# Attention probabilities turned by VectorE and carried through DRAM, instead of turned by TensorE

## The chip, the cores and the metric

The program runs on one core of one Trainium2 chip. The metric is the device time of one execution in microseconds (us), the median of three runs. In this document PE is TensorE (PEld its weight loads), ACT is ScalarE, DVE is VectorE, POOL is GpSimd and SP is SyncE, which does nothing here but issue DMAs.

## The reference

Three layers follow each other on a tensor of 4 batches, 576 tokens and 512 features, all in float32:

```
scores = q @ k.T / 8                      # 4 x 8 heads, 64 features each
keep 32 previous keys (heads 0-3) or every 4th of 128 previous keys (heads 4-7)
attn = exp(scores - max) / (sum + 1e-9);  x = attn @ v
xk, xr = mu * x + (1 - mu) * x_of_the_token_before         # two mixes
x = sigmoid(xr @ w_r) * (relu(xk @ w_k) ** 2 @ w_v)        # 512 -> 1024 -> 512
u = x + (token mix of rank 32 by U and V)
out = u + relu(u @ w_ch1) @ w_ch2                          # 512 -> 2048 -> 512
```

## The kernel before

**Attention in parts and pairs.** The 576 tokens of each batch are cut in two, 256 and 320, which makes eight parts (`k` = 0 to 7, the odd ones with 320 tokens). In each part the eight heads are worked as four pairs (`p` = 0 to 3; pairs 0 and 1 are dilated, 2 and 3 plain). `n = 4k + p` numbers all 32. One pair has four steps:

- A: DVE turns q and k, which DMAs have brought from DRAM, in 32x32 blocks.
- B: PE multiplies q by k into PSUM (L1300, L1313), DVE adds the mask and takes the maximum (L1052 to L1062), ACT takes the exponentials in place in `probs` (L766), four or five units of 64 queries by 64 or 96 keys.
- C: DVE divides by the sum (`normalise`, L1085 to L1090), PE turns the probabilities, one transpose for each unit (L1320), ACT copies the result from PSUM to `probs_t` (L756).
- D: PE multiplies `probs_t` by v (L1331), DVE copies the result into x (L1072 to L1076).

**Beside the second layer.** The second layer is worked in chunks of 256 tokens (`c` = 0 to 8), each chunk in ten slots. A slot is one unit of PE work on the mixed tokens: slots 0 to 3 and 6 to 9 hold the units k0 to k3 and k4 to k7 (12 matmuls of 256 columns), slots 4 and 5 the units r0 and r1 (12 matmuls of 512 columns). ACT takes relu and square of each k unit (`relu` L841, `high_sq` L846), and DVE takes the same square once more and the difference of the two (`square`, L1110 and L1114), because a product is done in three matmuls of high and low parts (L1279 to L1281). The down projection of a unit m, `values(c, m)`, waits for that difference `sq_l`. I call it v0 to v7: v0 in slot 3, v1 in slot 4, v2 in slot 5, v3 in slot 7, v4 in slot 8, and v5, v6 and v7 one after the other in slot 9.

**What sets the order.** Tables (`LATER` and its two relatives) give each step of each pair a slot of this sequence, written out before the run. In the steady state, counted in slots modulo ten, A stands at 3, 5, 8 and 0, B at 4, 6, 9 and 1, C at 8, 0, 3 and 5 and D at 9, 1, 4 and 6, for pairs 0 to 3. The steps of a part stand beside a chunk that is one and a half earlier. The squares are one slot late on DVE. Each engine works in its own order and waits on semaphores. ACT runs the exponentials of a B step one slot after it. The mix of the next chunk (`shift` on ACT, L798 to L807, `mix` on DVE, L1099) stands between them.

**Loads.** SP issues all loads in one order: v of a pair waits until D of the pair three before has run, q and k wait until A of the pair three before has run. In the first parts (`KEYS_BY_SCALAR`, seven pairs) ACT issues k instead of SP. Each of q and k is four DMAs a pair.

Of the kernel before, what the change touches and what calls it, by code (L numbers as in the profile page):

```python
# [21 lines left out]
F32 = mybir.dt.float32  # L22
# [40 lines left out]
KEYS_BY_SCALAR = [(0, 0), (0, 1), (0, 2), (1, 0), (1, 1), (1, 2), (1, 3)]  # L63
# [27 lines left out]

BEFORE = [("B", 0, 0), ("B", 0, 1), ("C", 0, 0), ("B", 0, 2), ("D", 0, 0), ("C", 0, 1), ("B", 0, 3), ("D", 0, 1), ("C", 0, 2),
# [7 lines left out]
SECOND_ONE = {"A": [-5, -4, -2, 0], "B": [-4, -3, -1, 1], "C": [-2, 0, 3, 5], "D": [-1, 1, 4, 6]}  # L100
SLOT_OF = {}
for k in range(1, NPART):
    for p in range(PAIRS):
        for st in "ABCD":
            n = (FIRST_ONE if k == 1 else SECOND_ONE if k == 2 else LATER)[st][p]
            if n is not None:
                SLOT_OF[st, k, p] = NUNIT * (k - 1) + n


def steps_in(slot):  # L110
    return sorted([step for step, n in SLOT_OF.items() if n == slot], key=lambda step: ("ACBD".index(step[0]), step[1:]))

# [69 lines left out]
SCALAR_SQUARES = [0] + list(range(MIX_CHUNK, NC1))  # L182
# [29 lines left out]
def build(nc, q, k_in, v, mu_k, mu_r, w_k, w_v, w_r, u_in, v_in, w_ch1, w_ch2, out):  # L212
    ctx = ExitStack()
    with ctx:
# [24 lines left out]
        probs_t = [sb(f"probs_t{n}", [UK, 5, P], c=first) for n in range(2)]  # L239
        mask_first = sb("mask_first", [P, 2, UK], BF16, c=first)  # L240
# [53 lines left out]
        sb("up_to_wr", [P, WPIECE], c=second)  # L294
# [11 lines left out]


# [22 lines left out]
        normed = sem("normed")  # L330
        carried = sem("carried")
# [113 lines left out]
        for n in range(NPART * PAIRS):  # L445
# [4 lines left out]
            V_COUNT.append(counts[RAWS + n % VALUES])  # L450

# [21 lines left out]
        def _(sp):  # L473
# [99 lines left out]
            for n in range(nth(2, 0), NPART * PAIRS):  # L573
                load_v(*divmod(n, PAIRS))
                if n + 2 < NPART * PAIRS:
                    load_qk(*divmod(n + 2, PAIRS))
                if n == nth(3, 0):
                    load_u()
                    load_piece(PIECE_V)
# [168 lines left out]
        def _(act):  # L748
# [21 lines left out]

            def attention_slot(slot):
# [5 lines left out]
                for k, p in behind:  # L777
                    exps(k, p, 1)

# [130 lines left out]

            def load_keys(k, p, parts=range(4)):
                n = nth(k, p)
                if n >= RAWS:
                    act.wait_ge(turned, n - RAWS + 1)
                for part in parts:
                    act.dma_start(raw_part(k_raw[n % RAWS], k, part), rows_of(k_in, k, p, part)).then_inc(qk_in[n % RAWS], 16)  # L916
# [90 lines left out]
        def _(dve):  # L1007
# [11 lines left out]
            def attention(stage_, k, p):  # L1019
# [23 lines left out]
                elif stage_ == "B":  # L1043

                    if n >= 2:
                        wait_mm(dve, ("C", *divmod(n - 2, PAIRS)))
# [45 lines left out]

            def mix(c, t):
# [12 lines left out]
            def square(c, m):  # L1106

                if c not in SCALAR_SQUARES:
# [3 lines left out]
                wait(dve, square_done, c * M1 + m + 1)  # L1112
# [161 lines left out]
        def _(pe):  # L1274
# [8 lines left out]
            def attention(stage_, k, p):  # L1283
# [37 lines left out]
                else:  # L1321
                    pe.wait_ge(values_in[n % VALUES], V_COUNT[n])
                    wait_drained(pe, ("C", k, p))
                    for i, (query, keys) in enumerate(every):
                        wide = BLOCK if dil and i == 4 else UQ
                        for a in range(UQ // wide):
                            for h in range(2):
                                rows = slice(DH * h, DH * h + DH)
                                block_, first = (4, DH * h + wide * a) if i == 4 else (2 * h + i // 2, UQ * (i % 2))
                                to = query + wide * a  # L1330
                                ins = pe.matmul(run[rows, to:to + wide], v_raw[n % VALUES][0:keys, i + a, rows],  # L1331
                                                probs_t[n % 2][0:keys, block_, first:first + wide], start=True, stop=True)
# [206 lines left out]
```

## Time and profile before

| | us |
|---|---|
| median of three runs | 762.47 (762.42 to 763.02) |
| the profiled execution's own time | 762.07 |
| its span in the profile | 760.0 |
| PE busy | 739.1 (97%) |
| DVE busy | 329.0 (43%) |
| ACT busy | 301.3 (40%) |
| POOL busy | 166.2 (22%) |

The profile is of one execution. Its span goes from the first to the last instruction, and about 2 us of the execution's own time lie around it. A matmul's recorded duration overlaps the next one, so what a group of matmuls costs is read from the starts of the instructions around it. PEclk, the granted clock of TensorE, is at its full value in all slices of the page.

### The profile page before, as it was taken

The numbers are of one execution on the slowest core, as the hardware profiler recorded it, in microseconds if no ns is written. First come the engines' busy times: TensorE is split into PE (matmuls) and PEld (weight loads), VectorE is DVE, ScalarE is ACT, GpSimd is POOL, SyncE is SP. The second block draws the span as 40 slices with busy tenths as digits, with TensorE's granted clock in tenths as the row PEclk, the third lists the DMA queues.
The fourth block names the chain that finished last, engine by engine and source line by source line (L and its number), as shares of the span: only waits on it lengthen the run. The fifth ranks groups of instructions, "written<-read, shape, count | busy, mean of one in ns | idle before, by whom it ended". The sixth has DMA issues, their size and how long they took to land.

```text
span 760.0 us, 13291 instructions
## 1 busy us (share of the span) xinstructions
PE 739.1 (97%) x4960; PEld 647.2 (85%) x4960; DVE 329.0 (43%) x695; ACT 301.3 (40%) x801; POOL 166.2 (22%) x257
## 2 busy tenths in 40 slices
PE   4799999999999999999999999999999999999998
PEld 3678888888888887888899989999999999899997
DVE  6888685868576746635321221312131131213111
ACT  4786767777777656635331111211111111112110
POOL 6897021202121133405871000000000000000000
PEclk9999999999999999999999999999999999999999
DMA  7864443333232101002342102100110210011001
GB/s 143 192 169 87 82 84 55 65 66 59 46 66 51 42 1 56 1 28 74 133 135 34 42 1 41 42 0 16 26 41 0 41 41 0 13 28 41 1 1 41
DMA packets 153746, 39.68 MB, mean 52 GB/s; under 512 B 141536, under 2 KB 147680, under 8 KB 153696
## 3 DMA queue, kind: packets, MB, share of 16 engines
q1 hardware_dynamic: 144000, 37.96, 21.5%
q10 hardware_dynamic: 9696, 1.05, 1.0%
q8 instruction: 31, 0.51, 0.3%
q14 instruction: 19, 0.16, 0.1%
HBM read 30.33 MB, written 4.72 MB: 46 GB/s over the span
## 4 chain that ended last, share of the span: by engine, by line
PE 94%; DVE 2%; ACT 1%; DMA 1%; issue 1%; POOL 0%; ACTq 0%; DVEq 0%
PE bank L1279 29%; PE bank L1281 28%; PE bank L1280 28%; PE bank L1331 3%; PE bank L1300 2%; PE bank L1320 2%; PE bank L1423 1%; PE bank L1435 1%; PE bank L1313 1%; POOL w_l L647 0%; ACTq L916 0%; DMA stage<-in_moe_w_ch_dram 0%; ACT probs L766 0%; DVE probs L1052 0%; DVE q_t L1030 0%
## 5 line engine op out<-in xcount | busy, mean ns | idle before, releaser
L1246 DVE SCALAR_TENSOR_TENSOR h_l<-bank,h_h 128x384 fp32r<-128x384 f32 x96 | 53.5, 558 | 288.1 <-ACT h_h L991 288.1
L991 ACT ACTIVATE h_h<-bank 128x384 fp32r<-128x384 f32 x96 | 47.1, 491 | 312.1 <-PE bank L1281 312.1
L1281 PE MATMUL bank<-ut_h,w_l 128*128 128x384 f32 x384 | 129.4, 337 | 0.0
L1279 PE MATMUL bank<-ut_h,w_h 128*128 128x384 f32 x384 | 129.3, 337 | 0.0
L1280 PE MATMUL bank<-ut_l,w_h 128*128 128x384 f32 x384 | 128.9, 336 | 0.0
L1281 PE MATMUL bank<-w_h,h_l 128*128 128x512 f32 x288 | 113.7, 395 | 0.0
L1280 PE MATMUL bank<-w_l,h_h 128*128 128x512 f32 x288 | 113.5, 394 | 0.0
L1279 PE MATMUL bank<-w_h,h_h 128*128 128x512 f32 x288 | 112.0, 389 | 0.0
L1279 PE MATMUL bank<-xs_h,wk_h 128*128 128x256 f32 x288 | 84.9, 295 | 0.2
L1280 PE MATMUL bank<-xs_l,wk_h 128*128 128x256 f32 x288 | 81.1, 282 | 0.0
L1281 PE MATMUL bank<-xs_h,wk_l 128*128 128x256 f32 x288 | 80.9, 281 | 0.0
L1279 PEld LDWEIGHTS bank<-ut_h,w_h 128*128 128x128 f32 x384 | 72.1, 188 | 4.6 <-issue 0.8
L1280 PEld LDWEIGHTS bank<-ut_l,w_h 128*128 128x128 f32 x384 | 72.1, 188 | 3.6
L1281 PEld LDWEIGHTS bank<-ut_h,w_l 128*128 128x128 f32 x384 | 72.0, 188 | 0.0
L1281 PEld LDWEIGHTS bank<-w_h,h_l 128*128 128x128 f32 x288 | 54.0, 187 | 11.5
L1280 PEld LDWEIGHTS bank<-w_l,h_h 128*128 128x128 f32 x288 | 54.0, 187 | 9.5
L1279 PEld LDWEIGHTS bank<-w_h,h_h 128*128 128x128 f32 x288 | 54.1, 188 | 9.0
L1279 PE MATMUL bank<-wv_h,sq_h 128*128 128x512 f32 x144 | 58.4, 405 | 0.0
L1279 PEld LDWEIGHTS bank<-xs_h,wk_h 128*128 128x128 f32 x288 | 54.8, 190 | 3.9 <-issue 1.4
L1281 PE MATMUL bank<-wv_h,sq_l 128*128 128x512 f32 x144 | 56.9, 395 | 0.0
L1280 PE MATMUL bank<-wv_l,sq_h 128*128 128x512 f32 x144 | 56.9, 395 | 0.0
L1280 PEld LDWEIGHTS bank<-xs_l,wk_h 128*128 128x128 f32 x288 | 54.9, 191 | 1.2
(120 smaller groups left out, 1183.9 us busy)
## 6 DMA issues: line engine op xcount, KB each, us to landing
stage<-in_moe_w_ch_dram SPq DMA_DIRECT2D x16, 512.0 KB, 3.3
out_dram<-result SPq DMA_DIRECT2D x18, 256.0 KB, 2.0
u_tile<-result SPq DMA_DIRECT2D x80, 48.0 KB, 2.0
q_raw<-in_q_dram SPq DMA_DIRECT2D x64, 40.0 KB, 2.1
q_raw<-in_q_dram SPq DMA_DIRECT2D x64, 32.0 KB, 2.0
v_raw<-in_v_dram SPq DMA_DIRECT2D x32, 64.0 KB, 2.4
k_raw<-in_k_dram SPq DMA_DIRECT2D x48, 40.0 KB, 2.1
k_raw<-in_k_dram SPq DMA_DIRECT2D x52, 32.0 KB, 2.0
```

Source lines behind the costliest of these rows:

```text
L991: act.activation(h_h[:, m % KRING, :], h_bank[m % 2][:, 0:C2], ACT.Relu).then_inc(hh_done, 1)
L1246: dve.scalar_tensor_tensor(h_l[:, m % KRING, :], h_bank[m % 2][:, 0:C2], 0.0, h_h[:, m % KRING, :].bitcast(F32), op0=ALU.max, op1=ALU.subt ...
L1279: pe.matmul(dst, lhs[0], rhs[0], start=start, stop=False)
L1280: pe.matmul(dst, lhs[0], rhs[1], start=False, stop=False)
L1281: return pe.matmul(dst, lhs[1], rhs[0], start=False, stop=stop)
L1300: ins = pe.matmul(dst[UQ * a:UQ * a + UQ, h, col:col + keys], q_t[n % 2][rows, query:query + UQ], k_t[p][rows, first_key:first_key + keys] ...
L1313: ins = pe.matmul(out_, q_t[n % 2][rows, query + wide * a:query + wide * a + wide], rhs, start=True, stop=True)
L1320: ins = pe.transpose(run[0:keys, i * P:i * P + P], probs[n % 2][:, keys * i:keys * i + keys], ident[:, :])
L1331: ins = pe.matmul(run[rows, to:to + wide], v_raw[n % VALUES][0:keys, i + a, rows], probs_t[n % 2][0:keys, block_, first:first + wide], sta ...
L1423: pe.matmul(g_bank[b % 2][rows, :].rearrange("p (a b) -> p a b", a=KT), u_pad[:, b % 2, slot, :], xcols(t * P, P), start=slot < 4, stop=sl ...
L1435: ins = pe.matmul(mix_bank[t % 2][:, :], vp[:, col:col + P], g_split[:, b, :], start=n == 0, stop=n == len(parts) - 1)
```

## The change

From pair 2 of part 2 on (n = 10 to 31, 22 pairs) step C is gone from PE and ACT. In its place is a step T, two slots after B. DVE normalises the pair and turns it in 32x32 blocks into a new tile `probs_blocks`; SP writes that tile to DRAM with one DMA and, one slot later, reads it back with one DMA for every 32 keys (two or three), in an order that completes the transpose. D waits for these DMAs and reads `probs_t` in another layout. For the same pairs ACT issues the four DMAs of k, after the second half of the exponentials. In chunks 1 to 6 the squares of units 1, 3, 4 and 6, which DVE took, are taken by ACT. SP's loads are issued slot by slot instead of pair by pair.

```diff
+MOVED_FROM = nth(2, 2)
+KEYS_BY_SCALAR = FIRST_KEYS + [divmod(n, PAIRS) for n in range(MOVED_FROM, NPART * PAIRS)]
@@ the table of slots
+        if nth(k, p) >= MOVED_FROM:
+            del SLOT_OF["C", k, p]
+            SLOT_OF["T", k, p] = SLOT_OF["B", k, p] + 2
-SCALAR_SQUARES = [0] + list(range(MIX_CHUNK, NC1))
+SCALAR_CHUNKS = [0] + list(range(MIX_CHUNK, NC1))
+SCALAR_SQUARES = [(c, m) for c in range(NC1) for m in range(M1) if c in SCALAR_CHUNKS or m in (1, 3, 4, 6)]
@@ SP
+            def probs_to_dram(k, p):
+                n, (nu, keys) = nth(k, p), blocks(k, p)
+                sp.wait_ge(probs_turned, n - MOVED_FROM + 1)
+                wait_mm(sp, ("D", *divmod(n - 2, PAIRS)))
+                sp.dma_start(probs_dram[n % 2][:, 0:nu * keys], probs_blocks[n % 2][:, 0:nu * keys]).then_inc(probs_out, 16)
+
+            def probs_from_dram(k, p):
+                n, (nu, keys) = nth(k, p), blocks(k, p)
+                sp.wait_ge(probs_out, 16 * (n - MOVED_FROM + 1))
+                rows = probs_dram[n % 2][:, 0:nu * keys].rearrange("(g j) (b x) -> b j g x", g=NBLOCK, x=BLOCK * nu)
+                for b in range(keys // BLOCK):
+                    sp.dma_start(moved_view(n, keys)[BLOCK * b:BLOCK * b + BLOCK, :, 0:BLOCK * nu], rows[b]).then_inc(probs_in[n % 2], 16)
+
+            for slot in range(UNIT["r", 1], LAST_SLOT + 2):
+                for k, p in pairs_in("T", slot):
+                    probs_to_dram(k, p)
+                for k, p in pairs_in("T", slot - 1):
+                    probs_from_dram(k, p)
+                for n in [nth(k, p) + VALUES for k, p in pairs_in("D", slot - 1)]:
+                    if nth(2, 0) <= n < NPART * PAIRS:
+                        load_v(*divmod(n, PAIRS))
+                for n in [nth(k, p) + RAWS for k, p in pairs_in("A", slot - 1)]:
+                    if n < NPART * PAIRS:
+                        load_qk(*divmod(n, PAIRS))
...
@@ ACT
                 for k, p in behind:
                     exps(k, p, 1)
+                for n in [nth(k, p) + RAWS for k, p in behind]:
+                    if MOVED_FROM <= n < NPART * PAIRS:
+                        load_keys(*divmod(n, PAIRS))
+                if (c, m) in SCALAR_SQUARES:
+                    act.activation(sq[:, m % 2, :], relu_k[:, m % 2, :], ACT.Square)
                 act.activation(sq_h[:, m % KRING, :], relu_k[:, m % 2, :], ACT.Square).then_inc(sqh_done, 1)
-                if c in SCALAR_SQUARES:
-                    act.activation(sq[:, m % 2, :], relu_k[:, m % 2, :], ACT.Square).then_inc(square_done, 1)
@@ DVE
+            def turn_probs(k, p):
+                n, (nu, keys) = nth(k, p), blocks(k, p)
+                dve.wait_ge(normed, n + 1)
+                if n - 2 >= MOVED_FROM:
+                    dve.wait_ge(probs_out, 16 * (n - 2 - MOVED_FROM + 1))
+                to = probs_blocks[n % 2][:, 0:nu * keys].rearrange("p (b i x) -> p i b x", i=nu, x=BLOCK)
+                dve.transpose(to, probs[n % 2][:, 0:nu * keys]).then_inc(probs_turned, 1)
...
+                    for k, p in pairs_in("T", slot + n):
+                        normalise(k, p)
+                        turn_probs(k, p)
@@ PE, step D
-                    wait_drained(pe, ("C", k, p))
+                    if moved(k, p):
+                        pe.wait_ge(probs_in[n % 2], PROBS_COUNT[n])
+                    else:
+                        wait_drained(pe, ("C", k, p))
...
+                                if moved(k, p):
+                                    to = to.rearrange("p (g x) -> p g x", x=BLOCK)
+                                    part = moved_view(n, keys)[:, first // BLOCK:(first + wide) // BLOCK, BLOCK * block_:BLOCK * block_ + BLOCK]
```

Line numbers in the pieces that follow are those of each program: L1320 before is L1402 after, and L1279 to L1281 are L1361 to L1363.

On PE, before, between v4 and the last k unit of an odd part's chunk (`wv_h`, `wv_l` are weights of the down projection, `xs_h`, `xs_l` the mixed tokens):

```order
L1280 MATMUL bank<-wv_l,sq_h 128x512
L1281 MATMUL bank<-wv_h,sq_l 128x512
L1320 MATMUL bank<-ident,probs 96x128 x5
L1279 MATMUL bank<-xs_h,wk_h 128x256
L1280 MATMUL bank<-xs_l,wk_h 128x256
L1281 MATMUL bank<-xs_h,wk_l 128x256
```

The same place on PE after the change:

```order
L1361 MATMUL bank<-wv_h,sq_h 128x512
L1362 MATMUL bank<-wv_l,sq_h 128x512
L1363 MATMUL bank<-wv_h,sq_l 128x512
L1361 MATMUL bank<-xs_h,wk_h 128x256
L1362 MATMUL bank<-xs_l,wk_h 128x256
```

The five transposes have gone and nothing has taken their place on PE.

On DVE, before, slot 8 and the start of slot 9 beside an odd part (L1110 and L1114 are the square and its low part, L1099 the mix, L1030 step A, L1052 to L1062 step B):

```order
L1110 TENSOR_TENSOR sq<-relu_k 128x256
L1114 TENSOR_TENSOR sq_l<-sq,sq_h 128x256
L378 COPY shifted<-zeros 128x1
L1099 SCALAR_TENSOR_TENSOR xf<-x,mu,shifted 128x256
L1030 STREAM_TRANSPOSE q_t<-q_raw 128x320
L1030 STREAM_TRANSPOSE k_t<-k_raw 128x320
L1110 TENSOR_TENSOR sq<-relu_k 128x256
L1114 TENSOR_TENSOR sq_l<-sq,sq_h 128x256
L1052 SCALAR_TENSOR_TENSOR probs<-bank,mask_unit 128x384
```

The same place on DVE after the change:

```order
L1189 TENSOR_TENSOR sq<-relu_k 128x256
L1193 TENSOR_TENSOR sq_l<-sq,sq_h 128x256
L410 COPY shifted<-zeros 128x1
L1178 SCALAR_TENSOR_TENSOR xf<-x,mu,shifted 128x256
L1155 TENSOR_SCALAR sums<-sums 128x5
L1157 RECIPROCAL inv<-sums 128x5
L1160 TENSOR_TENSOR probs<-probs,inv 128x480
L1170 STREAM_TRANSPOSE probs_blocks<-probs 128x5x3x32
L1098 STREAM_TRANSPOSE q_t<-q_raw 128x320
L1098 STREAM_TRANSPOSE k_t<-k_raw 128x320
L1193 TENSOR_TENSOR sq_l<-sq,sq_h 128x256
L1122 SCALAR_TENSOR_TENSOR probs<-bank,mask_unit 128x384
```

Four instructions, the division and the turn, have come in ahead of step A, and one of the two squares has gone.

On SP, before, the loads of a pair of part 5 (v, then q and k):

```order
L496 DMA v_raw<-in_v_dram 96x4x64 x2
L510 DMA v_raw<-in_v_dram 48x2x64 x4
L483 DMA q_raw<-in_q_dram 32x10x32 x4
L483 DMA k_raw<-in_k_dram 32x10x32 x4
```

On SP after the change, a pair's way through DRAM with the loads around it:

```order
L622 DMA probs_dram<-probs_blocks 128x480
L526 DMA q_raw<-in_q_dram 32x8x32 x4
L629 DMA probs_t<-probs_dram 32x4x160 x3
L543 DMA v_raw<-in_v_dram 64x5x64
L546 DMA v_raw<-in_v_dram 32x5x64
```

The four DMAs of k have left SP. The write, the q loads of another pair and the three reads follow each other in one queue.

## Rows read from the trace of the kernel before

**Rows 1.** Busy time by stage: stretch, its width, each engine, granted clock, DMA share

```profile
60.00:280.00 220.00, 220.00 (x2047) 189.56 (x2046) 153.37 (x375) 152.48 (x451) 47.29 (x73) 1.00 0.31 58
```

**Rows 2.** Waits of PE's weight loads, 60 to 280 us: total, times, longest

```profile
PEld bank L1279 <- DVE sq_l L1114: 0.3, 2, 0.2
```

**Rows 3.** Timeline of PE around three groups of transposes: start, duration, instruction

```profile
117.01 0.40 PE L1281 MATMUL bank<-wv_h,sq_l 128*128 128x512 f32 x1
117.40 0.72 PE L1320 MATMUL bank<-ident,probs 128*96 128x128 f32 x5
...
118.19 0.40 PE L1280 MATMUL bank<-wr_l,xs_h 128*128 128x512 f32 x1
...
162.89 0.60 PE L1320 MATMUL bank<-ident,probs 128*96 128x128 f32 x4
...
163.45 0.28 PE L1280 MATMUL bank<-xs_l,wk_h 128*128 128x256 f32 x1
...
171.93 0.71 PE L1320 MATMUL bank<-ident,probs 128*96 128x128 f32 x5
...
172.59 0.28 PE L1280 MATMUL bank<-xs_l,wk_h 128*128 128x256 f32 x1
172.71 0.28 PE L1281 MATMUL bank<-xs_h,wk_l 128*128 128x256 f32 x1
```

**Rows 4.** Timeline of ACT, slot 5 beside part 5, pair 0

```profile
164.34 0.58 ACT L756 ACTIVATE probs_t<-bank 96x512 f32<-96x512 f32 x1
164.82 0.36 ACT L766 ACTIVATE probs<-probs,neg_max 128x96 f32<-128x96 f32 x1
...
165.89 0.50 ACT L798 ACTIVATE shifted<-x,om 128x256 f32<-128x256 f32 x1
```

**Rows 5.** Timeline of DVE, slots 6 to 9 of that chunk

```profile
166.42 0.15 DVE L378 COPY shifted<-zeros 128x1 f32<-128x1 f32 x1 [3.95 <-ACT shifted L798]
...
169.85 0.17 DVE L1085 TENSOR_SCALAR sums<-sums 128x5 f32<-128x5 f32 x1
...
170.85 0.42 DVE L1110 TENSOR_TENSOR sq<-relu_k 128x256 f32<-128x256 f32 x1
171.30 0.42 DVE L1114 TENSOR_TENSOR sq_l<-sq,sq_h 128x256 fp32r<-128x256 f32 x1
...
172.66 0.47 DVE L1030 STREAM_TRANSPOSE k_t<-k_raw 128x320 f32<-128x320 f32 x1
...
174.83 0.56 DVE L1052 SCALAR_TENSOR_TENSOR probs<-bank,mask_unit 128x384 f32<-128x384 f32 x1 [0.93 <-PE bank L1313]
...
177.59 0.43 DVE L1114 TENSOR_TENSOR sq_l<-sq,sq_h 128x256 fp32r<-128x256 f32 x1
```

**Rows 6.** Timeline of PE: D of that pair, and v7

```profile
174.61 0.89 PE L1331 MATMUL bank<-probs_t,v_raw 96*64 96x64 f32 x24
...
178.33 0.40 PE L1279 MATMUL bank<-wv_h,sq_h 128*128 128x512 f32 x1
```

**Rows 7.** DMA issues of the page: count, size, us from issue to landing

```profile
out_dram<-result SPq DMA_DIRECT2D x18, 256.0 KB, 2.0
...
q_raw<-in_q_dram SPq DMA_DIRECT2D x64, 40.0 KB, 2.1
...
k_raw<-in_k_dram ACTq DMA_DIRECT2D x16, 40.0 KB, 3.3
```

**Rows 8.** Timeline of ACT and its DMA issues, early in the program

```profile
21.34 2.52 ACTq L916 DMA_DIRECT2D k_raw<-in_k_dram  x5
23.91 0.51 ACT L798 ACTIVATE shifted<-x,om 128x256 f32<-128x256 f32 x1 [2.21 <-DVE x L1072]
...
32.13 0.40 ACTq L916 DMA_DIRECT2D k_raw<-in_k_dram  x1
...
33.59 0.48 ACTq L916 DMA_DIRECT2D k_raw<-in_k_dram  x1
...
34.37 0.40 ACT L846 ACTIVATE sq_h<-relu_k 128x256 fp32r<-128x256 f32 x1
```

More of the change, by code:

```diff
@@ L180, with vector_squares @@
 MIX_CHUNK = NC1 - 2
-SCALAR_SQUARES = [0] + list(range(MIX_CHUNK, NC1))
+SCALAR_CHUNKS = [0] + list(range(MIX_CHUNK, NC1))
+SCALAR_SQUARES = [(c, m) for c in range(NC1) for m in range(M1) if c in SCALAR_CHUNKS or m in (1, 3, 4, 6)]
+def vector_squares(c, m):
+    return sum((a, b) not in SCALAR_SQUARES for a in range(c + 1) for b in range(M1) if (a, b) <= (c, m))
 LATE = 2 * NUNIT
@@ L239, in build @@
         probs_t = [sb(f"probs_t{n}", [UK, 5, P], c=first) for n in range(2)]
+        probs_blocks = [sb(f"probs_blocks{n}", [P, 5 * UK], c=first) for n in range(2)]
         mask_first = sb("mask_first", [P, 2, UK], BF16, c=first)
@@ L293, in build @@
         mix2_weights(3)
-        sb("up_to_wr", [P, WPIECE], c=second)
+        sb("up_to_wr", [P, WPIECE + 2 * 5 * UK], c=second)
         mix2_weights(1)
@@ L305, in build @@
         first_t_bank = [bank[0], bank[4], bank[1]]
+        probs_dram = [nc.dram_tensor(f"probs_dram{n}", (P, 5 * UK), F32, kind="Internal").ap() for n in range(2)]
         turned = sem("turned")
@@ L330, in build @@
         normed = sem("normed")
+        probs_turned = sem("probs_turned")
+        probs_out = sem("probs_out")
+        probs_in = [sem(f"probs_in{n}") for n in range(2)]
         carried = sem("carried")
@@ L450, in build, with moved_view @@
             V_COUNT.append(counts[RAWS + n % VALUES])
+        PROBS_COUNT, counts = {}, [0, 0]
+        for n in range(MOVED_FROM, NPART * PAIRS):
+            counts[n % 2] += 16 * (blocks(*divmod(n, PAIRS))[1] // BLOCK)
+            PROBS_COUNT[n] = counts[n % 2]
+        def moved_view(n, keys):
+            return probs_t[n % 2][0:keys, :, :].rearrange("p a b -> p (a b)").rearrange("p (g x) -> p g x", g=NBLOCK)
         def piece(n):
@@ L572, in _ @@
             load_piece(9)
[L573 to L577, printed above, removed]
+            load_qk(2, 2)
+            def probs_to_dram(k, p):
[20 more added lines that the diff above has]
+                        load_qk(*divmod(n, PAIRS))
+                if slot == 2 * NUNIT:
                     load_u()
@@ L769, in exps, with load_keys @@
                     ins.then_inc(exped, 1)
+            def load_keys(k, p, parts=range(4)):
+                n = nth(k, p)
+                if n >= RAWS:
+                    act.wait_ge(turned, n - RAWS + 1)
+                for part in parts:
+                    act.dma_start(raw_part(k_raw[n % RAWS], k, part), rows_of(k_in, k, p, part)).then_inc(qk_in[n % RAWS], 16)
             def attention_slot(slot):
@@ L909, in chunk @@
                     high_u(0)
[L911 to L916, printed above, removed]
             def first_exps(k, p):
@@ L1329, in attention @@
                                 block_, first = (4, DH * h + wide * a) if i == 4 else (2 * h + i // 2, UQ * (i % 2))
-                                to = query + wide * a
-                                ins = pe.matmul(run[rows, to:to + wide], v_raw[n % VALUES][0:keys, i + a, rows],
-                                                probs_t[n % 2][0:keys, block_, first:first + wide], start=True, stop=True)
+                                to, part = run[rows, query + wide * a:query + wide * a + wide], probs_t[n % 2][0:keys, block_, first:first + wide]
+                                if moved(k, p):
+                                    to = to.rearrange("p (g x) -> p g x", x=BLOCK)
+                                    part = moved_view(n, keys)[:, first // BLOCK:(first + wide) // BLOCK, BLOCK * block_:BLOCK * block_ + BLOCK]
+                                ins = pe.matmul(to, v_raw[n % VALUES][0:keys, i + a, rows], part, start=True, stop=True)
                 ins.then_inc(att_mm, 1)
```

17 lines of the change are left out of this document (12 added, 5 removed).

## The prediction, made before the changed kernel was run

> **What bounds the kernel now.** I read the page first, for the shares of the engines, then busy time by stage, then PE's waits, then the timelines of PE, ACT, DVE and SP over one chunk. In the stage that the change touches, 60 to 280 us, PE is busy for 220.00 of 220 us at full granted clock, while DVE has 153 us and ACT 152 us of work [rows 1]. The reader is to see that PE never stops there, so that whatever leaves PE shortens the program by its own length, unless another engine is then late. PE's waits in this stage are small. One of them names what would be late first: `sq_l`, the low part of a square, which DVE hands over just before v7 needs it [rows 2]. PE is busy 97% of the whole span, so I take it that a gain in this stage is carried to the end: all later work starts from PE's progress.
>
> **What leaves PE.** The price of a group of transposes is read from the starts around it. For five transposes, the second matmul after them starts at 172.59, 0.66 us after the group's start, and without the group it would start 0.12 after it, as its follower does: 0.54 us. For four: 163.45 - 162.89 - 0.12 = 0.44 us. In slot 3 of an odd part the group also costs a gap ahead of it: 118.19 - 117.01 is 1.18 us where two steps of 512 columns would stand, 0.24 each at the pace of the 256-column steps (0.12), so 0.70 us [rows 3]. The 22 moved pairs are 10 of even parts (four transposes) and 12 of odd parts (five), 3 of the latter in slot 3: 10 x 0.44 + 9 x 0.54 + 3 x 0.70 = 4.4 + 4.9 + 2.1 = 11.4 us. This is the gain if nothing is late.
>
> **What comes onto DVE.** The normalising moves, and the turn is new. The k_t row turns 320 elements in 0.47 us, which makes 0.70 for 480. The next instruction starts a little before such a record ends, so I take 0.65 us, between 0.4 and 1.1 (the second if the strided output made it half as long again). 22 turns, 4 of them of 256 and 6 of 384 elements, are some 13 us; 24 squares of 0.45 us (171.30 - 170.85) go, 11 us [rows 5]. On the whole DVE's load stays, and it has 67 us of idle time in 220. What counts is slots 6 to 9, where v7 stands at the end. I follow part 5, and the anchor is ACT: its shift starts at 165.89, 0.48 us earlier once the copy of C (164.34 to 164.82) is gone [rows 4]. DVE waits for it at 166.42, so it now starts at 165.94. Before, it needed from there to 177.59 + 0.43 = 178.02 for the `sq_l` of v7, 11.6 us, of which 0.93 us were a wait for PE's B [rows 5]. New in this stretch are two turns (1.3) and one more normalising (1.0, as 170.85 - 169.85); two squares go (0.9), and with DVE later than PE the wait of 0.93 goes too: 11.6 + 1.3 + 1.0 - 0.9 - 0.9 = 12.1, which ends at 178.05. PE has lost two groups in between (0.44 and 0.54) and comes to v7 at 178.33 - 0.98 = 177.35 [rows 3, 6]. So PE waits 0.7 us for v7, once for each odd part 3, 5 and 7: 2.1 us. With the bounds of the turn (0.4 and 1.1) it is 0.6 to 4.8 us in all. Beside the even parts 4 and 6 the same tiles are 256 wide instead of 480, and I count nothing. The wait is not added to other waits of the same slot: if D has waited just before, v7 waits less.
>
> **The way through DRAM.** The nearest rows are a store to DRAM, 2.0 us to landing, and a q load of 40 KB, 2.1 us; the slowest such median is 3.3 us, for k loads at the program's start [rows 7]. I take 2.1 for each of the two hops, the range is 2.0 to 3.3. The tightest pair is pair 0 of an odd part, turned in slot 6 and used in slot 9. DVE starts the division at about 166.5, turns until 168.2; SP issues the write at once, the four q loads take its queue for some 1.9 us, at 0.48 an issue [rows 8], the write has landed at 170.3, the three reads are issued from 170.7 at 0.5 us each, and the last lands at 171.7 + 2.1 = 173.8. PE comes to D at 174.61 - 0.98 = 173.6 [rows 6]. That is a wait of 0.2 us, and it lies inside the 0.7 already counted for v7. By the same steps pair 0 of an even part, with 256 columns and two reads, has about 1 us to spare, and the pair turned in slot 1 about 2; those turned in slots 3 and 8 have three slots of longer work before D, 3 us or more.
>
> The Trainium skill (DMA: Bandwidth & Descriptors, section Anatomy of one DMA) says that most of the fixed 2 us is the receipt from the target memory, and that the delay can be surprisingly long when the target is HBM. The store row of 2.0 us [rows 7] shows no such excess; if the rule held, the first hop would be longer and the first rival below would be the case. The same skill (VectorE: DVE Perf Modes, section Rules for kernel authors) advises TensorE for a 128x128 transpose whenever PSUM will do as its target. It speaks against this change outright. The rows speak for it, since here the engine that the rule spares is idle for 30% of the stage and the one that it uses is never idle [rows 1].
>
> **ACT.** It loses 22 copies (0.48 us here) and gets 24 squares of about the same length, which is even. It also issues 88 DMAs at 0.48 us, 1.95 us for each pair. Bounds: nothing, if they are issued while ACT's queued work runs, and 1.95 us a pair if ACT stands still. Both are seen. From 32.13 to 34.07 four are issued under five exponentials, and the next activation starts at 34.37 with no gap. From 21.34 five follow three others and ACT then idles 2.21 us [rows 8]. In the change four follow four or five exponentials, the first case, so I take nothing.
>
> **SP and D.** SP loses 88 issues and gets 22 writes and 62 reads, and it now waits twice a pair; q and v are loaded for three pairs ahead, tens of us, so a late issue costs nothing. D reads `probs_t` in runs of 32 columns, which I price at nothing. No wait for a bank is new, since C has left the two banks that the steps share.
>
> **The sum.** 762.07 - 11.4 + 2.1 = 752.8 us for the profiled execution, whose span would be 750.7 with the same 2.1 us around it; the median of the runs is 0.4 above it, so I predict 753.2 us. The spread of the runs is under 0.1%, and about 0.2%, 1.5 us, can be told from no change.
>
> **The rivals.**
>
> *The way back from DRAM is late.* If a hop takes x us longer, D waits 2x more. At x = 0.6 (a hop of 2.7 us) the pair in slot 9 beside an odd part waits 1.4 instead of the 0.7 that v7 counts already, 3 x 0.7 = 2.1 us more, and 0.2 in each of two even places: 755.7 us. At x = 1.1 it is 2.4 in the three places, 1.2 in the two even ones and 0.2 in the six of slot 1: 3 x 1.7 + 2.4 + 1.2 = 8.7 us more, 762 us. So this rival holds 755.5 to 762 and I price it at 758. For it: one queue, a write and reads with small runs, a slack near zero in one place. Against it: all medians of this stage are near 2 us.
>
> *Slower: ScalarE's issues of k hold it up.* Place: slots 5 and 7, ahead of the shifts on which DVE's mixes wait, as at 166.42 [rows 5]. If all 1.95 us of a pair stand open, DVE and v7 are that much later: 2 x 1.95 beside each of three odd parts (11.7), some 2 us beside each of two even ones (4), about 0.2 in slot 1 of six chunks, together 17 us against a net gain of 9.3: 770 us. The point from which it decides is 9.3 / 17 of 1.95, about 1.1 us left open a pair. For it: the row at 21.34. Against it: the row at 32.13, which has the same order of work as the change.
>
> *The full gain.* If the turn takes 0.4 us and DVE catches up, v7 waits 0.2 us or less: 762.5 - 11.4 + 0.6 = 751.7, and down to the bare 751.1. For it: PE's waits were nearly nothing before. Against it: the 12.1 us worked out above.
>
> **How the numbers follow.** The forecast, 751.8 to 755.5 us: 0.60. Late from DRAM, 755.5 to 762: 0.21, of which 0.04 within 0.2% of the median. Held up by ACT: 0.12, nearly all slower. The full gain, under 751.8: 0.07. Faster by over 0.2% is 0.60 + 0.17 + 0.07 = 0.84, within 0.2% 0.05, slower 0.11. The range of 750.5 to 760 leaves out the slower rival and the last part of the late one.
>
> **What will show it.** In the changed kernel's profile PE's matmuls should run without L1402 after about 70 us. PE should still be busy nearly all of 60 to 270. Its waits should name `sq_l` (L1193) in slot 9 beside odd parts, some 0.7 us each and 2 us in all, and `probs_t`'s DMA hardly at all. The turn L1170 should take 0.5 to 0.8 us, the two hops 2.0 to 2.3 us each. ACT should issue k with no gap in its activations. I am wrong if PE waits for DMAs of `probs_t` by more than 3 us in all, if ACT idles behind its own issues, or if D's matmuls (L1419) stand further apart than before.

## The result, and the profile after

The changed kernel takes 767.09 us (764.28 to 769.71, 10 runs), the kernel before 762.86 us beside it. The ratio is 1.0054, with a 95% interval of 1.0036 to 1.0072: slower by about 4 us, where 753.2 us was predicted. The profiled execution took 767.08 us, with a span of 765.2.

Busy time of the changed kernel over the same stretch as [rows 1], and in three windows of 5 us (columns as there):

```profile
60.00:280.00 220.00, 207.97 (x1915) 178.15 (x1914) 152.13 (x369) 146.69 (x445) 51.53 (x72) 0.98 0.45 99
...
105.00:110.00 5.00, 4.74 (x52) 4.03 (x53) 4.19 (x11) 1.83 (x4) 2.80 (x4) 0.66 0.48 125
250.00:255.00 5.00, 3.77 (x50) 3.16 (x51) 4.20 (x12) 2.69 (x4) 2.89 (x5) 0.80 0.45 123
255.00:260.00 5.00, 5.00 (x26) 4.25 (x26) 2.55 (x4) 0.00 (x0) 0.00 (x0) 0.86 0.22 49
```

PE, which never stopped before, now stops for 12.0 us, and its granted clock falls in places. The waits behind it, in the changed kernel from 60 to 290 us (total, times, longest), where before there was almost nothing [rows 2]:

```profile
PE bank L1382 <- DVE k_t L1098: 7.4, 5, 1.9
PE bank L1382 <- DVE k_t L1106: 2.7, 5, 1.1
PE bank L1361 <- DVE sq_l L1193: 1.9, 3, 0.7
```

10.1 of the 12.0 us are B waiting for step A, a wait that the prediction does not contain. The three waits for `sq_l` are those of v4 in slot 8 beside parts 3, 5 and 7. L1098 is `k_t` of pair 2, made in slot 8, L1106 that of pair 0, made in slot 3. DVE of the changed kernel beside part 5, from the mix of slot 6 to step A of slot 8, the place of [rows 5]:

```profile
169.17 0.15 DVE L410 COPY shifted<-zeros 128x1 f32<-128x1 f32 x1 [4.50 <-ACT shifted L873]
...
170.88 0.68 DVE L1170 STREAM_TRANSPOSE probs_blocks<-probs 128x480 f32<-128x480 f32 x1
...
175.60 0.15 DVE L410 COPY shifted<-zeros 128x1 f32<-128x1 f32 x1 [0.90 <-ACT shifted L873]
...
176.19 0.16 DVE L1155 TENSOR_SCALAR sums<-sums 128x5 f32<-128x5 f32 x1
...
177.31 0.68 DVE L1170 STREAM_TRANSPOSE probs_blocks<-probs 128x480 f32<-128x480 f32 x1
177.91 0.47 DVE L1098 STREAM_TRANSPOSE q_t<-q_raw 128x320 f32<-128x320 f32 x1
178.30 0.47 DVE L1098 STREAM_TRANSPOSE k_t<-k_raw 128x320 f32<-128x320 f32 x1
```

PE of the same kernel at the same place:

```profile
173.96 0.50 PE L1361 MATMUL bank<-wv_h,sq_h 128*128 128x512 f32 x1 [0.61 <-DVE sq_l L1193]
174.30 0.39 PE L1362 MATMUL bank<-wv_l,sq_h 128*128 128x512 f32 x1
174.53 0.39 PE L1363 MATMUL bank<-wv_h,sq_l 128*128 128x512 f32 x1
...
176.74 0.28 PE L1363 MATMUL bank<-xs_h,wk_l 128*128 128x256 f32 x1
178.92 0.56 PE L1382 MATMUL bank<-k_t,q_t 64*64 64x96 f32 x16 [1.90 <-DVE k_t L1098]
```

The mix waits 0.90 us for ACT's shift, T takes 176.19 to 177.91, and only then does DVE turn q and k; `k_t` is done at 178.77. The last record of PE ended at 177.02, and PE started B at 178.92. In the kernel before, `k_t` was begun at 172.66 [rows 5] and done at 173.13, and PE came to B here:

```profile
173.97 0.56 PE L1300 MATMUL bank<-k_t,q_t 64*64 64x96 f32 x16
```

So A had 0.84 us to spare. Both kernels can be counted from the mix of slot 6 (166.42 and 169.17). From there to the end of `k_t` DVE needs 6.71 us before and 9.60 us after, 2.89 us more: two T's (3.44) and the wait for the shift (0.90) have come in, one division (1.00) and one square (0.45) have gone. PE comes to B 7.55 us after that mix before and 7.85 us after the change, its wait for v4 included. 0.84 + 0.30 - 2.89 is 1.75 us too late, close to the 1.90 measured. T of pair 1 alone, which stands directly in front of A, is 1.72 us of it.

The hops through DRAM, to be held against [rows 7], on the page of the changed kernel:

```profile
probs_dram<-probs_blocks SPq DMA_DIRECT2D x12, 240.0 KB, 2.0
probs_t<-probs_dram SPq DMA_DIRECT2D x36, 80.0 KB, 2.2
k_raw<-in_k_dram ACTq DMA_DIRECT2D x64, 40.0 KB, 2.3
```

ACT and its issues of k in slot 5, which answer to [rows 4, 8]:

```profile
168.09 0.48 ACTq L841 DMA_DIRECT2D k_raw<-in_k_dram  x1
168.13 0.36 ACT L831 ACTIVATE probs<-probs,neg_max 128x96 f32<-128x96 f32 x1
...
168.62 0.51 ACT L873 ACTIVATE shifted<-x,om 128x256 f32<-128x256 f32 x1
```

The last of the four issues is shown; all four lie under the exponentials, and the shift follows with next to no gap.

**Where the time went.** I mark the stage by the first and the last of seven rows of DVE's `x<-bank,sig`, one for each chunk. In the kernel before:

```profile
72.28 1.29 DVE L1188 TENSOR_TENSOR x<-bank,sig 128x512 f32<-128x512 f32 x2 [0.15 <-PE bank L1281]
...
285.09 1.29 DVE L1188 TENSOR_TENSOR x<-bank,sig 128x512 f32<-128x512 f32 x2 [0.86 <-PE bank L1281]
```

and in the changed kernel:

```profile
72.45 1.29 DVE L1270 TENSOR_TENSOR x<-bank,sig 128x512 f32<-128x512 f32 x2
...
290.35 1.29 DVE L1270 TENSOR_TENSOR x<-bank,sig 128x512 f32<-128x512 f32 x2 [0.62 <-PE bank L1363]
```

The stage takes 217.9 us against 212.8. From its end on both kernels take the same (760.0 - 285.09 = 474.9, 765.2 - 290.35 = 474.9), and up to its start within 0.2 us. The difference of 5.1 us is made inside it. Five experiments below give the stage with less waiting. The table takes PE's recorded waits from the length of the stage.

| kernel | stage | PE waits | difference |
|---|---|---|---|
| e1 | 210.8 | 6.8 | 204.0 |
| e5 | 209.7 | 5.5 | 204.2 |
| e6 | 211.5 | 7.7 | 203.8 |
| e9 | 205.5 | 0.7 | 204.8 |
| e10 | 207.0 | 3.7 | 203.3 |

Net of the recorded waits the stage is 8.8 us (8.0 to 9.5) shorter than the 212.8 us of the kernel before. That is not the price of C, because a wait costs more than its record. A record of PE ends 0.16 us after the next matmul could have started (0.28 us long, at a step of 0.12), and the wait is counted from that end; and behind the wait ahead of 173.96 above the next matmul stands 0.34 us later instead of 0.23. In e5 the steps with its 13 gaps take 2.3 us more than the gaps' records, and the steps behind them 0.6 us more.

Summed from start to start in the same stage, this has left PE: the 100 transposes (9.15 us), the slow first step behind each group (1.85) and the gap ahead of the three groups in slot 3 (0.47), together 11.5 us. For e9, in which nothing is turned, this closes: 212.8 - 11.5 + 1.4 of gaps + 2.7 in the steps at and behind them = 205.4, for 205.5. In the changed kernel the 38 steps begun at the lower clock are 3.0 us longer than such steps are at full clock, and 212.8 - 11.5 + 12.0 of waits + 2.2 in the steps around them + 3.0 = 218.5, for 217.9. The 0.6 us are open.

### The profile page after: what moved, and what is told of

It reads as the page before. It is cut to its first block, busy times and chain, and to the rows that moved or that the text cites. A ratio compares the mean times of both kernels' runs of the same rounds, so it can differ in the third digit from the quotient of the medians.

```text
span 765.2 us, 13125 instructions
## 1 busy us (share of the span) xinstructions
PE 732.6 (96%) x4860; PEld 640.9 (84%) x4860; DVE 328.7 (43%) x693; ACT 299.2 (39%) x803; POOL 172.0 (22%) x257
## 3 DMA queue, kind: packets, MB, share of 16 engines
q10 hardware_dynamic: 36704, 4.34, 3.7%
## 4 chain that ended last, share of the span: by engine, by line
PE 77%; ACT 9%; DVE 8%; issue 3%; ACTq 2%; DMA 1%; POOL 0%; DVEq 0%
PE bank L1361 24%; PE bank L1363 24%; PE bank L1362 24%; ACT probs L831 4%; ACTq L841 2%; PE bank L1419 2%; PE bank L1382 2%; DVE probs L1160 1%; DVE q_t L1098 1%; ACT L831 1%; ACT shifted L873 1%; DVE xf L1178 1%; PE bank L1510 1%; DVE neg_max L1132 1%; DVE probs L1122 1%
## 5 line engine op out<-in xcount | busy, mean ns | idle before, releaser
L1363 PE MATMUL bank<-ut_h,w_l 128*128 128x384 f32 x384 | 129.5, 337 | 0.0
L1361 PE MATMUL bank<-ut_h,w_h 128*128 128x384 f32 x384 | 129.3, 337 | 0.0
L1363 PE MATMUL bank<-w_h,h_l 128*128 128x512 f32 x288 | 113.7, 395 | 0.0
L1361 PE MATMUL bank<-w_h,h_h 128*128 128x512 f32 x288 | 112.0, 389 | 0.0
L1361 PE MATMUL bank<-xs_h,wk_h 128*128 128x256 f32 x288 | 83.8, 291 | 0.2
L1363 PE MATMUL bank<-xs_h,wk_l 128*128 128x256 f32 x288 | 81.1, 282 | 0.0
L1361 PEld LDWEIGHTS bank<-ut_h,w_h 128*128 128x128 f32 x384 | 72.2, 188 | 4.5 <-issue 0.8
L1363 PEld LDWEIGHTS bank<-ut_h,w_l 128*128 128x128 f32 x384 | 72.0, 188 | 0.0
L1363 PEld LDWEIGHTS bank<-w_h,h_l 128*128 128x128 f32 x288 | 54.0, 188 | 11.5
L1361 PEld LDWEIGHTS bank<-w_h,h_h 128*128 128x128 f32 x288 | 54.2, 188 | 9.0
L1361 PE MATMUL bank<-wv_h,sq_h 128*128 128x512 f32 x144 | 59.7, 415 | 1.9 <-DVE sq_l L1193 1.9
L1361 PEld LDWEIGHTS bank<-xs_h,wk_h 128*128 128x128 f32 x288 | 55.0, 191 | 4.6 <-issue 1.4
L1363 PE MATMUL bank<-wv_h,sq_l 128*128 128x512 f32 x144 | 57.9, 402 | 0.0
L797 POOL COPY u_tile<-x 128x512 f32 (+1 forms) x15 | 8.8, 616 | 214.8 <-DVE ut_l L1226 214.8
```

The source lines that it names most:

```text
L797: pool.tensor_copy(u_tile[:, :, t * P:t * P + P], xcols(c * C2 + t * P, P))\
L1361: pe.matmul(dst, lhs[0], rhs[0], start=start, stop=False)
L1363: return pe.matmul(dst, lhs[1], rhs[0], start=False, stop=stop)
```

## The experiments

**e1: step A ahead of T** (in slots 8 and 3).

```diff
-                    for k, p in pairs_in("T", slot + n):
+                    late = any(step[0] == "A" for step in steps_in(slot + n))
+                    for k, p in pairs_in("T", slot + n) if not late else []:
                         normalise(k, p); turn_probs(k, p)
 ...                 attention(*step)
+                    for k, p in pairs_in("T", slot + n) if late else []:
+                        normalise(k, p); turn_probs(k, p)
```

> Step A goes ahead of step T on VectorE in slots 8 and 3, nothing else. Theory (order): the changed kernel lost its gain because T, 1.7 us of VectorE, stands ahead of A, and PE's next scores (B) wait for A: 10.1 us of PE's 12.0 us of waits. Then those waits fall to under 2 us, the granted clock stays full, and the time is 752 to 756 us. Rival (load): VectorE has too much to do in slots 6 to 9 whatever the order; then the waits move to the low part of the square or to B's drain, PE still idles 6 us or more, and the time stays above 760 us. Rival (DRAM): T is now up to 1.2 us later, and D waits for the probabilities from DRAM instead, over 3 us in all.

759.93 us, ratio 0.9961 (0.9937 to 0.9985). PE's waits from 60 to 290 us:

```profile
PE bank L1365 <- DVE sq_l L1193: 5.7, 8, 1.0
PE bank L1423 <- DMA probs_t<-probs_dram: 0.6, 1, 0.6
PE bank L1386 <- DVE k_t L1098: 0.5, 2, 0.2
```

The wait for A goes from 10.1 to 0.5 us and the kernel becomes 7.2 us faster than the changed one: the order of T and A on DVE is the cause of those waits. The time is 4 us above what I expected, though, and what the rival on DVE's load said is met in part: PE still idles 7.0 us, 5.7 of them for `sq_l`, which is next in DVE's queue.

**e5: step A ahead of the mix as well** (and so always ahead of T).

```diff
+                    steps = steps_in(slot + n) if c < MIX_CHUNK else []
+                    for step in steps:
+                        if step[0] == "A":
+                            attention(*step)
                     for t in range(KT): ...mix...
                     for k, p in pairs_in("T", slot + n): ...
-                    for step in steps_in(slot + n) if c < MIX_CHUNK else []:
-                        attention(*step)
+                    for step in steps:
+                        if step[0] != "A":
+                            attention(*step)
```

> On VectorE step A goes ahead of the mix and of T in its slot (in e1_a_first it went ahead of T only). In e1_a_first PE still waited 5.7 us for the low part of squares, in two places: for v4, whose sq_l stands behind B and D of slot 6, and for v7 beside odd parts, at the end of a chain in which VectorE idles 0.9 us for ScalarE's shift just ahead of the mix of slot 8. Theory (chain): A, 0.8 us, fills that idle time, v7's wait of 0.9 us beside each of three odd parts goes, v4's stays: 757 us. Rival (load): the work counts and not its place, 760 us as in e1_a_first.

758.89 us, ratio 0.9948 (0.9931 to 0.9965). PE's waits:

```profile
PE bank L1366 <- DVE sq_l L1193: 4.1, 6, 0.9
PE bank L1424 <- DMA probs_t<-probs_dram: 1.4, 3, 1.0
```

A now runs while DVE would stand for ACT's shift. No wait for `k_t` is left. The step from e1 to e5, 1 us, is within the two intervals.

**e2: are the waits dearer than their length?** PE fills most of its wait ahead of B of pair 2 with multiplications of the identity, whose result nobody reads.

```diff
                 if stage_ == "B":
+                    if k >= 3 and p == 2:
+                        for _ in range(8 if half else 4):
+                            pe.matmul(run[:, 0:P], ident[:, :], ident[:, :], start=True, stop=True)
                     wait(pe, turned, n + 1)
```

> The changed kernel with idle matmuls (identity by identity, 128 columns, float32) on PE ahead of the scores of pair 2 in slot 9: eight in odd parts, four in even ones, where PE waits 0.8 to 1.9 us. They write where the scores are written afterwards. Theory (clock): PE's waits stand, but the granted clock stays at its full level after them, and the 4 to 5 us that separate the changed kernel from the sum of its own terms come back: about 763 us, with a spread under 1 us instead of 5. Rival: the clock falls for another reason (load, DMA), and the time is that of the changed kernel, 767, or more by the matmuls' own time.

765.64 us (764.71 to 768.35), ratio 1.0031 (1.0015 to 1.0047): 1.5 us faster than the changed kernel and not the 763 us with a small spread that I expected. 9 of its 12 runs had a mean granted clock of 1.0, of the changed kernel's ten none. Its profiled execution shows what the others avoid, after a wait of 2.19 us that was not filled:

```profile
155.00:160.00 5.00, 2.81 (x45) 1.96 (x44) 3.69 (x11) 3.88 (x8) 1.24 (x2) 0.98 0.56 136
160.00:165.00 5.00, 5.00 (x23) 3.95 (x22) 2.98 (x8) 0.28 (x1) 0.00 (x0) 0.68 0.43 82
```

That idle PE costs a second time through the clock is likely from this and not shown. The two intervals overlap, so the 1.5 us are a sign and not a measured price. And the clock also falls in a kernel whose profiled execution has no wait of PE in this stage: of 22 repeats of the kernel before, in the same round of runs, 6 had a mean clock of 0.995 or 0.996 and 765.9 to 767.2 us, the others at most 764.0 us. Only a repeat at full clock was profiled, so where the clock fell in those is not known.

**e3: the 24 squares back on DVE.**

```diff
-SCALAR_SQUARES = [... if c in SCALAR_CHUNKS or m in (1, 3, 4, 6)]
+SCALAR_SQUARES = [... if c in SCALAR_CHUNKS]
```

> The changed kernel with the squares of units 1, 3, 4 and 6 on VectorE again, as before (24 more instructions of 0.45 us there, as many fewer on ScalarE). Theory (order): VectorE is the engine that is late in slots 8 and 9, and each square ahead of A (units 4 and 5 or 6, 0.45 us each) adds to PE's wait: 0.45 to 0.9 us in each of five chunks, 3 to 5 us more than the changed kernel, 770 to 772 us. Rival (ScalarE is what is late): the squares off ScalarE shorten its chain by 0.33 us each and the time falls below 767.

767.52 us, ratio 1.0048 (1.0029 to 1.0067): the same as the changed kernel, where I expected 3 to 5 us more. PE waits for `k_t` as long as there (10.0 us) and for `sq_l` 1.4 us longer:

```profile
PE bank L1361 <- DVE sq_l L1193: 3.3, 3, 1.1
```

So moving these squares gained nothing in an order in which B waits for T.

**e4: k issued by SP again.**

```diff
-KEYS_BY_SCALAR = FIRST_KEYS + [divmod(n, PAIRS) for n in range(MOVED_FROM, NPART * PAIRS)]
+KEYS_BY_SCALAR = FIRST_KEYS
@@ ACT, behind the exponentials
-                        load_keys(*divmod(n, PAIRS))
```

> The changed kernel with k issued by SP again, in one go with q. Theory (order): ScalarE's issues were hidden under its exponentials (its idle time behind them is 4.1 us in all over five places), so their going gives little, under 1.5 us; SP's four more issues, 1.9 us, stand between the write to DRAM and the reads in slots where q of a later pair is loaded, so the probabilities come up to 1.9 us later and D waits in slot 9 beside odd parts: together 765 to 769 us. Rival (ScalarE's issues were the cause): PE's waits for A vanish and the time falls to 755 to 760 us.

786.15 us, ratio 1.0305 (1.0278 to 1.0332), 19 us slower than the changed kernel and far outside what I expected. SP of this kernel, from the write of pair 0 to its reads:

```profile
100.68 0.38 SPq L622 DMA_DIRECT2D probs_dram<-probs_blocks  x1
101.10 1.96 SPq L526 DMA_DIRECT2D q_raw<-in_q_dram  x4
103.10 1.93 SPq L526 DMA_DIRECT2D k_raw<-in_k_dram  x4
105.07 2.67 SPq L629 DMA_DIRECT2D probs_t<-probs_dram  x3
```

and its PE:

```profile
PE bank L1416 <- DMA probs_t<-probs_dram: 14.2, 8, 3.9
```

The reads are ready when the write has landed, at 102.7, and stand 2.4 us behind q and k. PE waits 21.4 us in all, 9.4 more than in the changed kernel, and the clock falls more often too (mean 0.984 over the span, 0.995 in the changed kernel). The profiled execution is 14.8 us longer; how the rest beyond the 9.4 us divides between the clock and the steps around the waits I did not work out.

**e7: k by ACT and the squares on ACT, with C on PE as before.**

```diff
-MOVED_FROM = nth(2, 2)
-KEYS_BY_SCALAR = ... range(MOVED_FROM, ...)
+MOVED_FROM, KEYS_FROM = NPART * PAIRS, nth(2, 2)
+KEYS_BY_SCALAR = ... range(KEYS_FROM, ...)
```

> The two side edits alone: k issued by ScalarE from pair 10 on and the 24 squares on ScalarE, with the probabilities turned by TensorE as before. Theory (order): PE is never late in the kernel before, so neither edit can gain; ScalarE's issues are hidden under exponentials; 762.5 to 763.5 us. Rival (ScalarE's issues): PE waits and the time is over 765 us.

763.25 us, ratio 1.0004 (0.9984 to 1.0023), no change. Busy time of that kernel:

```profile
60.00:280.00 220.00, 219.90 (x2046) 189.48 (x2045) 144.54 (x352) 159.80 (x476) 46.40 (x73) 1.00 0.31 57
```

Beside a PE that is never late, ACT's issues of k and its squares cost nothing that can be told within 0.2%.

**e9: nothing is turned.** The order of e5 without the turn and both hops; D multiplies by old probabilities.

```diff
                     for k, p in pairs_in("T", slot + n):
                         normalise(k, p)
-                        turn_probs(k, p)
@@ DVE, mask of B
-                        dve.wait_ge(probs_turned, n - 2 - MOVED_FROM + 1)
+                        dve.wait_ge(normed, n - 1)
@@ SP
-                for k, p in pairs_in("T", slot): probs_to_dram(k, p)
-                for k, p in pairs_in("T", slot - 1): probs_from_dram(k, p)
@@ PE, D
-                    if moved(k, p):
-                        pe.wait_ge(probs_in[n % 2], PROBS_COUNT[n])
```

> This is e5's order with the turning and both hops through DRAM left out (D multiplies by an old probs_t that nobody fills again, so the outputs are wrong there; 22 turns on DVE, 22 writes and their reads are missing, the normalising stays). Theory (C's removal is worth about 10 us, and the rest of the 11.4 us of the prediction's step 1 is not idle time but a price that was put too high): TensorE has next to no wait between 60 and 280 and the time is 752.5 to 754.5, that is e5's 758.9 less its 5.5 us of waits. Theory 2 (removal worth the full 11.4 us, and something beside the waits slows TensorE in e5, such as the DMA traffic): 751 to 752. Theory 3 (the clock falls whatever is done once C is gone, because the engine is still fed unevenly): above 755.

755.06 us (752.68 to 757.74, only 4 runs), ratio 0.9884 (0.9838 to 0.9930). The granted clock was 1.0 in three of the four. Busy time from 60 to 280 us:

```profile
60.00:280.00 220.00, 218.58 (x1986) 185.75 (x1986) 153.72 (x358) 154.22 (x465) 58.96 (x81) 1.00 0.31 58
```

This is about what the removal of C can give in this order: between 5 and 12 us by the interval, and 7.3 us in the stage of the profiled execution. The four runs decide nothing between the theories: 755.06 us is 0.6 above the first, at the edge of the third, whose falling clock is not seen in three of them, and the 751 to 752 us of theory 2 lie inside the interval of the ratio. The steps of PE (above) speak for theory 2: 11.5 us have left, and what slows PE beside the recorded waits lies in the steps at and behind nine short stops.

**e6: an early square.** e5 with the square of unit 4 ahead of B and D in slot 6, since v4 waits for it.

```diff
+EARLY = [(c, 7) for c in range(1, MIX_CHUNK - 1)]
...
-                    if n >= 1 and UNITS[n - 1][0] == "k":
+                    if n >= 1 and (c, n) not in EARLY and UNITS[n - 1][0] == "k":
                         square(c, UNITS[n - 1][1])
...T...
+                    if (c, n + 1) in EARLY:
+                        square(c, UNITS[n][1])
...B, D...
```

> As e5_a_before_mix, and the low part of square 4 goes ahead of B and D of slot 6, in chunks 1 to 5. Theory (chain): v4's wait, 0.6 to 1.0 us in each of five chunks, goes too, PE idles under 1.5 us between 60 and 280 us, and the time is 753 to 754.5 us, which is what the prediction's sum gives without its term for v7 (751.5) plus a small rest: the term for the removed transposes, 11.4 us, is then right. Rival: removed transposes are worth less than 11.4 us, for the part that other matmuls hide; then PE does not wait and the time is still above 756 us.

761.45 us, ratio 0.9979 (0.9963 to 0.9995): 2.6 us slower than e5, where I expected 753 to 754.5 us. PE of e6 at D of pair 0, and its waits in all:

```profile
104.31 0.89 PE L1427 MATMUL bank<-probs_t,v_raw 96*64 96x64 f32 x24 [1.94 <-DMA probs_t<-probs_dram]
```

```profile
PE bank L1427 <- DMA probs_t<-probs_dram: 4.9, 5, 1.9
PE bank L1369 <- DVE sq_l L1194: 2.8, 3, 1.5
```

The wait moved from `sq_l` to `probs_t`. SP of e6:

```profile
97.16 0.34 SPq L623 DMA_DIRECT2D probs_dram<-probs_blocks  x1
97.55 2.83 SPq L527 DMA_DIRECT2D q_raw<-in_q_dram  x4
100.42 1.40 SPq L630 DMA_DIRECT2D probs_t<-probs_dram  x3
```

and of e5 at the same place:

```profile
95.44 0.34 SPq L622 DMA_DIRECT2D probs_dram<-probs_blocks  x1
95.82 1.99 SPq L526 DMA_DIRECT2D q_raw<-in_q_dram  x4
97.86 1.41 SPq L629 DMA_DIRECT2D probs_t<-probs_dram  x3
```

Counted from the write, PE of e5 starts D with next to no wait 6.1 us later (101.57). PE of e6, no longer held at v4, is there after 5.2 us (104.31 - 1.94 - 97.16), and the reads are issued 0.84 us later than in e5, since q's four issues took that much longer. 0.9 sooner and 0.84 later, with 0.2 for a slower landing, are the 1.94 us. So the wait at v4 had covered the way through DRAM. Why the sum of the waits, 7.7 us, is more than e5's 5.5 beyond this one place I did not trace.

**e8: e6 and the squares of units 5 and 7 on ACT.**

```diff
-... or m in (1, 3, 4, 6)]
+... or m in (1, 3, 4, 5, 6, 7)]
```

> As e6_early_square, with the squares of units 5 and 7 on ScalarE too, where it idles 1.5 us for the maximum and 5.6 us for the next chunk. Theory: VectorE is the last to arrive in slot 9 by less than 0.5 us; if anything of v7's wait was left, it goes: 752.5 to 754 us, at most 1 us under e6_early_square. Rival: ScalarE's later shift or high part puts off the mix, and it is the same or up to 1 us slower.

759.19 us, ratio 0.9951 (0.9932 to 0.9970), as fast as e5 and 5 us above what I expected. Of its 6.0 us of waits 4.7 are for `probs_t`:

```profile
PE bank L1427 <- DMA probs_t<-probs_dram: 4.7, 4, 1.8
```

**e10: e5 with the same six squares on ACT, without the early one.** The edit is that of e8, on e5.

> e5's order and squares of m = 5 and 7 on ScalarE as well, without the early square of e6. Theory (e6 lost because square 4's low part stood ahead of B on VectorE, which made the exponentials, ScalarE's shift, the mix, T and so the landing of probs_t late; what was gained at v4 was paid at D): with two of VectorE's squares gone and nothing put ahead of B, waits for sq_l beside odd parts fall from 4.1 to about 2 us, those for probs_t stay at about 1.4, and the time is 757.0 (756.3 to 758.0). Rival (e8's result came from the early square, and the squares on ScalarE only load the engine that the shift waits for): 759 to 761, with probs_t waits above 3 us.

757.89 us, ratio 0.9919 (0.9891 to 0.9948), the fastest version that does all the work, though its interval overlaps with e5's.

```profile
PE bank L1366 <- DVE sq_l L1193: 2.0, 3, 0.7
PE bank L1424 <- DMA probs_t<-probs_dram: 1.7, 3, 0.8
```

The waits came as the theory had them: `sq_l` from 4.1 to 2.0, `probs_t` as in e5. The early square is what cost time in e6, and it gained nothing in e8. By which path it made the reads late (the exponentials, the shift and the mix, as I expected) was seen only in the one place above.

**e11: e10 with the reads issued straight after the write**, ahead of v and q.

```diff
-                for k, p in pairs_in("T", slot - 1):
+                for k, p in pairs_in("T", slot):
                     probs_from_dram(k, p)
```

> e10 with SyncE issuing the reads from DRAM right behind the write, ahead of q's and v's transfers (in the kernel before this edit q's four issues of 2.0 to 2.8 us stand between them). Theory (the last 1 to 2 us of waits at D come from SyncE's queue): no wait for probs_t's DMA between 60 and 290, and the time is 1.0 to 1.5 us under that of e10. Rival (q comes late instead, since SyncE now stands 2.1 us for the write to land before it issues q): VectorE waits for q_raw ahead of A, TensorE for k_t, and the time is 1 us or more above e10's.

758.89 us, ratio 0.9939 (0.9918 to 0.9961), not faster than e10. PE's waits:

```profile
PE bank L1424 <- DMA probs_t<-probs_dram: 2.9, 2, 2.5
```

Neither theory holds. Waits for `probs_t` became fewer (2 for 3) but one grew to 2.5 us, no q came late, and the waits for `sq_l` stayed at 2.0 us. The long wait stands at D at 123.48. Its pair was turned at 113.63, but SP was issuing the loads of U and V of the token mix (`u_pad`, `stage`) until 117.1 and issued the write at 117.23, and that write landed only after 2.84 us. So in this place what stands ahead of the write costs time, which neither theory had. In e10 too the time left to gain there is under 2 us.

## Why the prediction was wrong, step by step

- **PE's waits. This step failed.** The prediction followed DVE's queue through slots 6 to 9 and compared its end with PE at two places, D and v7. At B of slot 9 it found DVE "later than PE" and took 0.93 us of DVE's waiting away, but it put nothing in for PE, which then waits at B for `k_t`. It never compared `k_t` with B there, nor `k_t` with B in slot 4. A stands behind T in DVE's queue, had 0.84 us to spare and came 2.89 us later. Over both slots B waited 10.1 us, of which e1 takes all but 0.5 away. B waiting for step A is in no term of the sum. The row `k_t` stood in [rows 5]; with PE's row of B (173.97) the slack can be read.
- **The wait for `sq_l`.** 2.1 us were predicted, three waits of 0.7; 1.9 us, three waits of up to 0.7, were measured. That they agree is luck: all three are those of v4 in slot 8, which the prediction did not look at, and none is v7's. PE had by then been held by B, so v7 found its square ready.
- **What leaves PE.** 11.4 us were predicted, and 11.5 us left by the steps of PE from start to start. The size was right. What the sum lacked is that short stops cost PE 2 to 3 us beyond their recorded length (3.0 us in e5), so that a stage net of its recorded waits is only 8.8 us shorter.
- **The turn.** 0.65 us were predicted for 480 elements. The record is 0.68 us, and the next instruction starts 0.60 us after it (177.31 to 177.91).
- **DRAM.** The hops take 2.0 and 2.2 us in the median (2.1 predicted), and PE never waits for `probs_t` in the changed kernel. Three of the 22 writes landed only after 3.66 to 4.34 us, in slots with time to spare. But PE was late itself. Once B no longer waits, D waits 1.4 us (e5) to 4.9 us (e6). The times of this rival (755.5 to 762 us) hold those of e5, e6 and e8, but with medians near 2 us its slow hop is not what made D wait. The slow receipt that the prediction weighed is told of transfers that GpSimd issues, and here SP issues them.
- **ACT.** Nothing was predicted for k's issues and the squares. e7 bears it out where PE is never late. But a sign of being wrong is there: in the changed kernel ACT idles behind its issues in five places, once 1.87 us at 61.5 us and four times 0.47 to 0.67 us beside even parts, 4.1 us in all (1.0 us in two places in e7). The rival of 770 us wanted 1.1 us a pair and falls. Whether the four gaps lengthen B's waits of 0.81 and 1.02 us beside even parts no run separates.
- **SP.** "A late issue costs nothing" is not true for the reads. For pair 0 they land 0.8 to 2.6 us before D in the changed kernel, so that with 1.9 us of k in front of them (e4) the kernel is 19 us slower.
- **D and the carry to the end.** D's matmuls stand as far apart as before where the clock is full (16.0 us for the 440 of the stage, before and in e5), and 474.9 us follow the stage in both kernels. Both steps were right.
- **The clock.** It was not thought of. Full speed was taken as given, since PE was always busy. In the changed kernel it costs about 3 us. In the kernel before, the repeats with a clock of 0.995 or 0.996, about one in four, are some 3 us longer than its median.

## What to carry to other kernels

When work is put into an engine's queue, list everything behind it up to the next place where that engine idles, and compare each item with the moment at which its reader comes, not only the last item and the one that waited before. An engine that never waits has many tight hand-overs that its waits don't show; take their slack from the timeline (when the data was made, when the reader started). And count a short stop of PE at more than its recorded length: here 0.16 us more in the step itself, and about 0.1 us in the step behind it. Put what another engine waits for ahead of what only a DMA waits for: this exchange alone (e5) turned 0.5% slower into 0.5% faster.

## What the hardware did that I had not expected

TensorE's granted clock fell after short waits, though PE was 97% busy over the span before and 95% busy in this stage after (207.97 of 220 us). After the wait of 1.90 us that ended at 105.26 in the changed kernel, in a window of 5 us in which PE was busy for 3.06 us, the next 5 us were granted 0.66. In that stretch the 512-column matmuls follow each other at 0.43 us:

```profile
108.13 0.63 PE L1363 MATMUL bank<-wv_h,sq_l 128*128 128x512 f32 x1
108.56 0.63 PE L1361 MATMUL bank<-wv_h,sq_h 128*128 128x512 f32 x1
```

instead of the 0.23 us of 174.30 to 174.53 above. 0.43 to 0.23 is near the ratio of the two levels, 2.4 and 1.2 GHz. Of the three waits of 1.8 to 1.9 us in the changed kernel two are followed by this, those that ended at 105.26 and 251.24. After the third, at 178.92, the granted clock stays at 1.00, though PE was busy for only 3.10 us between 175 and 180, and it stays there behind the waits of 1.94 us in e6 and 1.82 us in e8. And repeats of one kernel differ in it: the changed kernel's runs have mean clocks of 0.993 to 0.998 and times of 769.7 to 764.3 us roughly in that order. The kernel before does it too, in 6 of 22, 7 of 34 and 3 of 13 repeats, all at 0.995 or 0.996, although its profiled execution has no wait of PE in this stage. What decides it stays open.
